# Sparse attention, a Sinkhorn-weighted expert layer and an ELU layer on one core: the order of products and down tiles within a unit

## The reference, cut to what matters

```
x = attention(q, k, v)                      # 4 x 576 tokens, 8 heads of 64 -> x: 2304 x 512
P = exp(x @ w_gate - max); 8 Sinkhorn steps # P: 2304 x 8 (rows, then columns, normalised in turn)
y = sum over e of P[:, e] * (relu(x @ w1[e]) @ w2[e])      # 8 experts, w1[e]: 512 x 1024
out = elu(y @ w_in) @ w_out                                # w_in: 512 x 2048
```

## Time and profile before

| | |
|---|---|
| median of 3 runs | 2138.15 us (2137.84 to 2145.97) |
| the profiled execution | 2146.04 us, span 2144.3 us |
| granted TensorE clock, mean | 0.983 of 2.4 GHz |
| TensorE busy (matmuls) | 2060.5 us, 96% of the span |
| VectorE busy | 1486.8 us, 69% |
| GpSimd busy | 1050.5 us, 49% |
| ScalarE busy | 930.3 us, 43% |

### The profile page before, as it was taken

One profiled execution on the slowest core, in us unless ns is written; L12 is line 12 of the kernel. 1 busy time (PEld: TensorE's weight loads), 2 busy tenths in 40 slices (PEclk: granted clock), 3 DMA queues, 4 the chain that ended last, 5 costly groups with the idle time before them and its releaser, 6 DMA issues.

```text
span 2144.3 us, 29144 instructions
## 1 busy us (share of the span) xinstructions
PE 2060.5 (96%) x10611; PEld 1842.8 (86%) x10611; DVE 1486.8 (69%) x2478; ACT 930.3 (43%) x1702; POOL 1050.5 (49%) x797
## 2 busy tenths in 40 slices
PE   5889998999999999999999999999999999999999
PEld 4878887998998889999899888898999899888888
DVE  3665887666666666666666778766666666678887
ACT  5883332333333433333333476533333333376675
POOL 2354543545454465454545546465454545546442
PEclk9988998999999999999999999999999999999999
DMA  7441111212122122221222211222221222211211
GB/s 142 94 81 40 59 59 41 78 59 79 59 71 68 59 71 68 63 76 60 79 59 72 66 60 59 89 74 65 67 71 60 79 60 74 65 60 60 89 60 58
DMA packets 159549, 147.64 MB, mean 69 GB/s; under 512 B 64688, under 2 KB 126384, under 8 KB 159408
## 3 DMA queue, kind: packets, MB, share of 16 engines
q1 hardware_dynamic: 159408, 145.79, 23.4%
HBM read 141.05 MB, written 4.72 MB: 68 GB/s over the span
## 4 chain that ended last, share of the span: by engine, by line
PE 81%; DVE 10%; ACT 5%; issue 3%; SPq 2%; DMA 0%; POOL 0%; DVEq 0%
PE psum L689 13%; PE psum L688 13%; PE psum L687 13%; PE psum L628 13%; PE psum L631 12%; PE psum L630 12%; DVE acc L1067 1%; DVE x_lo_a L986 1%; PE psum L562 1%; PE psum L586 1%; DVE prob L1083 1%; DVE w_lo L991 1%; DVE row_sum L1078 1%; PE psum L603 1%; SPq L382 1%
## 5 line engine op out<-in xcount | busy, mean ns | idle before, releaser
L480 POOL TENSOR_TENSOR w_lo<-w_raw,w_hi 128x1024 fp32r<-128x1024 f32 x120 | 294.4, 2453 | 934.0 <-ACT w_hi L816 934.0
L1067 DVE SCALAR_TENSOR_TENSOR acc<-psum,prob,acc 128x512 f32<-128x512 f32 x516 | 387.2, 751 | 291.9 <-PE psum L689 286.2
L689 PE MATMUL psum<-w_hi,h_lo 128*128 128x512 f32 x1440 | 570.5, 396 | 0.0
L688 PE MATMUL psum<-w_lo,h_hi 128*128 128x512 f32 x1440 | 568.7, 395 | 0.0
L687 PE MATMUL psum<-w_hi,h_hi 128*128 128x512 f32 x1440 | 566.8, 394 | 0.6 <-issue 0.6
L628 PE MATMUL psum<-x_hi_a,w_hi 128*128 128x384 f32 x1296 | 443.3, 342 | 22.7 <-DVE c L1024 20.7
L631 PE MATMUL psum<-x_hi_a,w_lo 128*128 128x384 f32 x1296 | 440.1, 340 | 0.0
L630 PE MATMUL psum<-x_lo_a,w_hi 128*128 128x384 f32 x1296 | 438.8, 339 | 0.0
L689 PEld LDWEIGHTS psum<-w_hi,h_lo 128*128 128x128 f32 x1440 | 272.3, 189 | 59.7
L687 PEld LDWEIGHTS psum<-w_hi,h_hi 128*128 128x128 f32 x1440 | 273.4, 190 | 47.8 <-issue 0.9
L688 PEld LDWEIGHTS psum<-w_lo,h_hi 128*128 128x128 f32 x1440 | 272.6, 189 | 47.9
(11 more groups left out here) (115 smaller groups left out, 2838.7 us busy)
## 6 DMA issues: line engine op xcount, KB each, us to landing
w_raw<-in_moe_w_dram SPq DMA_DIRECT2D x192, 512.0 KB, 3.6
w_raw<-in_moe_w_in_dram SPq DMA_DIRECT2D x24, 512.0 KB, 3.4
w_raw<-in_moe_w_out_dram SPq DMA_DIRECT2D x24, 512.0 KB, 3.7
v_l<-in_v_dram SPq DMA_DIRECT2D x24, 128.0 KB, 3.7
out_dram<-acc SPq DMA_DIRECT2D x2, 1536.0 KB, 6.1
raw_l_q<-in_q_dram SPq DMA_DIRECT2D x16, 144.0 KB, 3.4
raw_l_k<-in_k_dram SPq DMA_DIRECT2D x16, 144.0 KB, 4.0
raw_s_q<-in_q_dram SPq DMA_DIRECT2D x16, 144.0 KB
```

What stands on the lines that cost most here:

```text
L480: pool.tensor_tensor(w2_lo[n % 2][:, :, :], w2_raw[:, :, :], w2_hi[n % 2][:, :, :].bitcast(f32), ALU.subtract).then_inc(w2_lo_s, 1)
L688: pe.matmul(dst, h_hi[:, i, kk, js], w2_lo[s][:, i, :], start=False, stop=False)
L689: mm = pe.matmul(dst, h_lo[:, i, kk, js], w2_hi[s][:, i, :], start=False, stop=(i == 1))
L1067: ins = dve.scalar_tensor_tensor(a, y, 1.0 if bare else gate_of(n, j), a, ALU.mult, ALU.add)
```

## The change

Only orders change; no instruction is added or taken away. On TensorE the tiles d0 to d5 now stand between the products:

before: p1 p6 p5 d0 d1 d2 p2 p7 d3 p4 d4 d5 p3

after: p1 p6 d0 p5 d1 d2 p2 d3 p7 d4 p4 d5 p3

`turn_back` stays behind d0, d1 and d2, `sum_columns` behind d2. On VectorE the split of w1 stands ahead of `make_u2` in every body. With an ELU unit u, `make_u2` and `evict(u, 0)` stand ahead of `elu_sum(E12)`, where they stood behind it or behind `elu_lo(H12)`. Eviction 3 stands ahead of `make_u3`, eviction 4 ahead of `make_c21`, and in ELU units `elu_sum(E21)` behind eviction 5. The orders of ScalarE, GpSimd and the DMA queue are the same.

```diff
             for u in range(U):
...
                 if more:
                     p1(n)
                     p6(n)
+                down(u, 0)
+                if js_y:
+                    turn_back(p_y, js_y[0])
+                if more:
                     p5(n)
-                for j in range(HT):
-                    down(u, j)
-                    if j < len(js_y):
-                        turn_back(p_y, js_y[j])
+                down(u, 1)
+                if js_y:
+                    turn_back(p_y, js_y[1])
+                down(u, 2)
+                if js_y:
+                    turn_back(p_y, js_y[2])
                 if u < SINKHORN_STEPS:
                     sum_columns(u)
                 if more:
                     p2(n)
+                down(u, 3)
+                if more:
                     p7(n)
-                down(u, HT)
+                down(u, 4)
                 if more:
                     p4(n)
-                down(u, HT + 1)
-                down(u, HT + 2)
+                down(u, 5)
                 if more:
                     p3(n)
...
-                if n + 1 < U and u >= 0 and is_elu(u):
+                if n + 1 < U:
                     split_w1_a(n + 1)
-                if u >= 0 and is_elu(u):
-                    elu_sum(u, E12, c12[u % 2][:, :], c12[u % 2][:, :])
-                    evict(u, 0)
-                    elu_lo(u, H12, c12[u % 2][:, :])
                 if more:
                     make_u2(n)
-                if n + 1 < U and not (u >= 0 and is_elu(u)):
-                    split_w1_a(n + 1)
+                if u >= 0 and is_elu(u):
+                    evict(u, 0)
+                    elu_sum(u, E12, c12[u % 2][:, :], c12[u % 2][:, :])
+                    elu_lo(u, H12, c12[u % 2][:, :])
...
-                    make_u3(n)
-                    make_c22(n)
-                    if is_elu(n):
-                        elu_sum(n, E11, elu[E11][:, :], bank(W)[:, 0:HTOK])
                 if u >= 0:
                     evict(u, 3)
                 if more:
                     if is_elu(n):
+                        elu_sum(n, E11, elu[E11][:, :], bank(W)[:, 0:HTOK])
+                    make_u3(n)
+                    make_c22(n)
+                    if is_elu(n):
                         elu_lo(n, H11, elu[E11][:, :])
-                    make_c21(n)
-                    if is_elu(n):
-                        elu_sum(n, E22, c22[:, :], c22[:, :])
                 if sink is not None:
                     sink_cols(sink)
                 if u >= 0:
                     evict(u, 4)
                 if more:
+                    make_c21(n)
                     if is_elu(n):
-                        elu_sum(n, E21, c21[:, :], c21[:, :])
+                        elu_sum(n, E22, c22[:, :], c22[:, :])
                     else:
                         relu_lo(n, H21, c21[:, :])
                 if u >= 0:
                     evict(u, 5)
                 if more and is_elu(n):
+                    elu_sum(n, E21, c21[:, :], c21[:, :])
                     elu_lo(n, H21, c21[:, :])
```

## The result

The changed kernel takes 2215.35 us (median of 4 runs, 2213.57 to 2222.61) against 2142.06 us (4 runs, 2137.84 to 2148.82): 1.0345 times the time, with a 95% interval of 1.0305 to 1.0386. That is some 73 us slower; the forecast was 2220, from 2180 to 2240. The profiled execution took 2213.57 us, its span is 2211.8. Medians in this document are over all runs; ratios leave out three slow ones, one of the hybrid (2673 us) and two of the kernel before (2266 and 4513 us).

What follows compares the result with a forecast made beforehand. TensorE was taken to bound the kernel, busy throughout ReLU units, with ELU units becoming a longer cross-engine chain. ELU units +81, clock +4, late splits -3 gave +82 on 2138: 2220 us, range 2180 to 2240.

Steps and rivals of the forecast that it cites:

- ReLU units at no cost: In 96 of 120 units TensorE stays busy with the same matmuls; a steady unit stays 15.55 us, cost zero.
- Three things late in ELU units: In ELU units d0's wait for `elu_lo(H21)`, `make_c21` behind eviction 4, and `elu_sum(E12)`, the worst, come late.
- `elu_sum(E12)` behind GpSimd: VectorE's sum in ELU units, shut out by GpSimd's split of w2: start at c+4.86, end at c+7.01.
- c: Start of `make_c12(u)` on VectorE in an ELU unit, the zero point of the forecast's times.
- D: Start of TensorE's tile d3 in a clean ELU unit, forecast at c+8.25.
- The unit of 18.6 us: A clean ELU unit, without splits of the next pass's x: 8.25 + 10.34 = 18.6 us, against 15.75.
- The other ELU units: Nine units around each ELU pass, walked by kind, 187.1 us in sum: +31 us around pass 2, +30 around pass 4.
- The clock, +4: Four TensorE gaps of 3 us and more lower the granted clock: estimated +4 us, bounds zero and +15.
- (A): Rival: faster, as the new order covers every `make_u3` and `make_u2` and gaps shrink; 2103 or 2126 us; 5%.
- (C): Rival: no change within 0.5%, as the delays fit into waits on ScalarE; 4%.
- (B): Rival: chain exists but GpSimd doesn't shut out `elu_sum(E12)`; D = c+7.05, about +48 us for ELU units, 2187; 12%.
- (D): Rival: the forecast with more half-speed stretches from recurring idle times in each ELU unit, up to 2240 us; 14%.

Runs made afterwards that it cites:

- the hybrid: Kernel before, with both new orders only in bodies where both units are ReLU and old orders in every body with an ELU unit: 2132.17 us, ratio 0.9977.
- d0 fourth: Changed kernel with tile d0 put back behind p5 on TensorE in every body: 2217.36 us, 1.0372 times the kernel before.
- TensorE's order alone: Kernel before with the new TensorE loop and VectorE's old order: 2153.64 us, 1.0077 times the kernel before.
- the sum first: Changed kernel with `elu_sum(E12)` back ahead of `make_u2` and `evict(u,0)` in ELU bodies: 2170.49 us, 1.0164 times the kernel before.
- GpSimd swapped: Changed kernel with GpSimd splitting the sums of w1 before w2 in ELU bodies: 2181.33 us, 1.02 times the kernel before.
- VectorE's order alone: Changed kernel with the whole TensorE loop of the kernel before, VectorE's new order kept: 2420.5 us, 1.1323 times the kernel before.

## Why the prediction was right, point by point

**ReLU units at no cost.** Right but for a small term. TensorE was busy all the time, but one of the prediction's own signs of being wrong did come: ReLU units lengthened, by 0.05 us, which over some 80 is 4 us that the sum did not have. It goes with how often TensorE turns from products to tiles or back in a unit. With 6 turns (before) units 36 to 59 take 15.61 us each, with 8 (d0 fourth) 15.64, with 10 (after, and TensorE's order alone) 15.67: 0.01 us for each turn. Why a turn costs this is not shown. The 15.55 us of the prediction came from a count of matmuls in a window; the starts of `snap` give 15.60 to 15.64. The gain at late splits was forecast at 0.7 us each: the wait of the earlier trace rows fell from 2.16 to 1.30, and that of the rescaling unit from 8.8 to 2.9 + 3.5, which made this one unit 2.2 us shorter (27.4 to 25.2).

**Three things late in ELU units.** `elu_sum(E12)` behind GpSimd: forecast to start at c+4.86 and end at c+7.01, it ran from c+4.76 to c+6.97. D was forecast at c+8.25 and is c+8.18. The experiments with the sum first (39 us less) and with GpSimd swapped (31 us less) show it. The rule of the Trainium skill that the prediction cites ("SBUF — State Buffer", the two separate sides: the one of the two engines that starts second is blocked for the other's whole instruction) agrees with the 2.21 us, and with the 0.55 us once GpSimd is idle. `make_c21` behind eviction 4: shown, 0.6 us each. d0 as the third item on TensorE: it does wait, but in the changed kernel the wait costs nothing of its own ("d0 fourth"); what the TensorE order costs is that p7 and so `make_u3` come later, by 0.89 us. The waits before d0 and d3 were forecast at 1.1 and 1.9 us and at some 50 us in all; the trace has 0.42, 1.48 and 43. Part of that is how idle time is counted: from the modelled end of the matmul before, 0.34 to 0.39 us after its start, where the next one otherwise starts after 0.17 to 0.23.

**The unit of 18.6 us** was 18.1. From D to the next `make_c12` I had 10.34 us; it was 2127.83 - 2117.91 = 9.92. Half of the difference is `elu_lo(H11)`, which GpSimd held less than before: the step to eviction 4 was 0.56 us and not 0.78 (2122.79 to 2123.35). Besides, eviction 4 was followed after 0.60 us and not 0.68 (2123.35 to 2123.95), and `elu_lo(H11)` came 1.56 after `make_c22` and not 1.68 (ScalarE's copy followed its relu by 0.43 and not 0.53).

**The other ELU units.** The nine units around each ELU pass, us from `snap` to `snap`:

| unit | forecast | group 0 | group 1 |
|---|---|---|---|
| first | 15.7 | 18.0 | 18.0 |
| two with `turn_back`, each | 22.4 | 23.7, 23.8 | 24.6, 24.3 |
| three with one `split_x`, each | 20.9 | 20.4, 19.9, 20.4 | 20.4, 19.9, 20.4 |
| two x differences | 20 | 19.7 | 19.7 |
| three `split_x` | 23.2 | 23.3 | 23.3 |
| after the pass | 20.7 | 17.3 | 19.9 |
| sum | 187.1 | 186.4 | 190.5 |

The first units, for which the prediction shows no walk, were under-sized by 2.3 us, and the units with `turn_back` by 1.3 to 2.2; those with one `split_x`, the ones after the pass and the clean ones were over-sized. That the total for the ELU passes, +78 us and 2.3 in the tail against +81, came out so near is in part luck. With `turn_back` the second transposes did wait until c+9.06, as forecast (c+9.15). But I called this a gap of 3 us, which my own times contradict: TensorE is there at c+0.15 plus two tiles, a product and the first transposes, c+4.3, so nearly 5 us; it was 4.38 on the matmul row. And 1.2 GHz then fell on d2, inside the chain (window above, 0.57).

**The clock, +4.** The granted clock in the two middle stretches went from 0.99 and 0.98 to 0.96 and 0.94. From these, an estimate of the work lost to the lower clock is 0.03 x 186.4 + 0.04 x 190.5, some 13 us at most; how much of it lies in the chain is not shown, so the +4 is neither shown nor refuted. The mean over the whole is 0.983 in both profiles, because the Sinkhorn stretch had fewer slow parts in this one: four of its units took 19.3 us and the others 17.7 before (the granted clock is 0.91 in unit 3 and 1.00 in unit 4), and only one took 19.2 after. That is 5 us which the change did not bring, and a good part of why the two profiled executions differ by only 67.5 us while the ELU passes and the tail alone are 80 us longer; another 5 us lie ahead of unit 1. The waits of 1.1 and 1.9 us (0.4 and 1.5 by the trace) in clean units did not bring the clock down: 1.00 over all six.

**Rivals.** (A) and (C) fell with the time. What the prediction said for (A) of the Trainium skill ("Perfetto Trace Analysis", Optimization Strategy: interleaving regimes may improve performance) found nothing to work on here, where both regimes are TensorE's. (B), `elu_sum` not shut out, fell with the row of 2.21 us; but its number was near: with the cause taken away the kernel took 2181 us, against 2187 for (B). Its D of c+7.05 is a slip in the sum: `elu_sum` ending at c+5.4 with the same 1.24 us behind it gives c+6.64, and the run with GpSimd swapped has c+6.53 (in it the sum ended at c+5.32). (D) did not come.

**What I had wrong among the expectations** was the one for VectorE's order alone: I walked the ELU unit and forgot that the ReLU unit has the same pair, eviction 3 ahead of `make_u3`.

## What to carry to other kernels

An order on one engine is only as good as the last link behind it: before tiles are put between products, walk the cross-engine chain of each kind of unit once round, from an operation to the same one a unit later. If that period is longer than the bound engine's own time, the order loses, wherever the visible wait stands; and taking away the first wait (here d0) gave nothing. Reorderings of two engines are to be tried together and apart: one alone cost 13%.

Look at what each moved VectorE operation will run beside on GpSimd. Here swapping two GpSimd instructions, with no change to any other engine, was worth 31 us in the changed kernel; with the old orders around ELU units it brought clean units from 15.75 to 15.6 us, which is TensorE's own time.

## What the runs showed of the hardware that I had not expected

An `elu_sum` with both operands in SBUF was held for up to 1.7 us (2.23 against 0.56), though its shortest time, 541 ns, is no shorter than that of the form with a PSUM operand. That form, in the same kernel, never was held: it took 0.54 to 0.55 us in all 24 cases, 19 of them beside a running GpSimd operation. In the eleven traces here a VectorE operation of 128x384 with both operands in SBUF (`elu_sum`, `elu_lo` or `relu_lo`) started inside a GpSimd operation, with over 0.15 us of it left, 488 times, and each time it ended 0.40 to 0.43 us after that operation's end. The forms of L1015, min, median and max in ns:

```profile
L1015 DVE SCALAR_TENSOR_TENSOR c<-c,elu x72: 541/558/2226, 1223.8 to 2201.9; 128x384 f32<-128x384 f32 x72
L1015 DVE SCALAR_TENSOR_TENSOR elu<-psum,elu x24: 540/546/550, 1219.5 to 2190.8; 128x384 f32<-128x384 f32 x24
```

Four more turns between products and down tiles lengthened a gapless unit by 0.05 us in 15.6. Two waits in each unit, of 0.4 and 1.5 us, for 108 us left TensorE's granted clock at 1.00 (2.4 GHz), while the wait of 4.38 us was followed by 1.2 GHz for most of 4 us.
